# Outputs of a pair in one TensorE visit with the next pair's scores

## What is computed

```
# attention, for each batch and head
for t in range(768):
    state = alpha[t][:, None] * state + outer(k[t], v[t])   # 48 x 48
    y[t] = q[t] @ state
x = y, tokens as rows, heads side by side                    # 3072 x 384
x = square(relu(x @ w_in)) @ w_out                           # first layer
out = silu(x @ w2_in) @ w2_out                               # second layer
```

## Time and profile before

| | |
|---|---|
| median of 3 runs | 881.98 us (881.14 to 882.66) |
| profiled execution: time | 877.95 us |
| its span, first to last instruction | 876.3 us |
| TensorE matmuls busy | 862.5 us, 98% |
| VectorE busy | 541.2 us, 62% |
| ScalarE busy | 437.0 us, 50% |
| GpSimd busy | 104.2 us, 12% |
| granted TensorE clock, mean | 1.000 of 2.4 GHz |

### The profile page before, as it was taken

One profiled execution on the slowest core, in us unless ns is written; L12 is line 12 of the kernel. 1 busy time (PEld: TensorE's weight loads), 2 busy tenths in 40 slices (PEclk: granted clock), 3 DMA queues, 4 the chain that ended last, 5 costly groups with the idle time before them and its releaser, 6 DMA issues.

```text
span 876.3 us, 17615 instructions
## 1 busy us (share of the span) xinstructions
PE 862.5 (98%) x6834; PEld 707.5 (81%) x6834; DVE 541.2 (62%) x1072; ACT 437.0 (50%) x770; POOL 104.2 (12%) x127
## 2 busy tenths in 40 slices
PE   6999989999999999999999999999999999999998
PEld 6777768788878788788888888888888888888898
DVE  7788876777767667664334556556754446766620
ACT  5765544455446445544666744445434436554510
POOL 3453300000000000000354003003030003000000
PEclk9999999999999999999999999999999999999999
DMA  8885434333333332300412352000130000110010
GB/s 171 229 236 126 99 67 120 74 76 103 71 81 87 102 79 67 103 20 13 149 43 71 61 113 78 0 1 1 46 100 0 1 1 1 36 37 1 1 48 28
DMA packets 134203, 60.03 MB, mean 69 GB/s; under 512 B 81824, under 2 KB 129312, under 8 KB 134112
## 3 DMA queue, kind: packets, MB, share of 16 engines
q1 hardware_dynamic: 130800, 58.14, 26.9%
q10 hardware_dynamic: 3312, 0.69, 0.4%
HBM read 45.02 MB, written 9.44 MB: 62 GB/s over the span
## 4 chain that ended last, share of the span: by engine, by line
PE 93%; DVE 4%; issue 1%; ACT 1%; DMA 0%; DVEq 0%; ACTq 0%
PE z_ps L1146 21%; PE h_ps L1132 21%; PE h_ps L1175 20%; PE z_ps L1211 11%; PE jobs L1211 7%; PE jobs L1231 3%; PE jobs L1007 1%; PE jobs L1040 1%; PE jobs L1109 1%; DVE decay L1703 1%; PE jobs L1018 1%; PE jobs L1117 1%; PE h_ps L1231 1%; DVE decay L1688 1%; PE z_ps L1078 0%
## 5 line engine op out<-in xcount | busy, mean ns | idle before, releaser
L1429 ACT ACTIVATE g<-h_ps 128x512 f32<-128x512 f32 x96 | 57.4, 598 | 177.5 <-PE h_ps L1132 175.4
L1523 ACT ACTIVATE sum<-sum 128x512 f32<-128x512 f32 x96 | 60.6, 631 | 137.2 <-DVE sum L1871 111.9
L1810 DVE TENSOR_TENSOR g_lo<-g,g_hi 128x512 fp32r<-128x512 f32 x96 | 67.6, 705 | 85.4 <-ACT g L1435 85.3
L1871 DVE TENSOR_TENSOR sum<-h_ps,sum 128x512 f32<-128x512 f32 x120 | 83.0, 691 | 57.1 <-PE h_ps L1175 54.4
L1132 PE MATMUL h_ps<-x_hi,win_hi 128*128 128x512 f32 x288 | 115.0, 399 | 1.2 <-ACT g L1429 0.8
L1146 PE MATMUL z_ps<-g_hi,wout_hi 128*128 128x512 f32 x282 | 114.4, 406 | 0.0
L1132 PE MATMUL h_ps<-x_hi,win_lo 128*128 128x512 f32 x288 | 112.4, 390 | 0.0
L1132 PE MATMUL h_ps<-x_lo,win_hi 128*128 128x512 f32 x288 | 112.2, 389 | 0.0
L1146 PE MATMUL z_ps<-g_hi,wout_lo 128*128 128x512 f32 x282 | 110.2, 391 | 0.0
L1146 PE MATMUL z_ps<-g_lo,wout_hi 128*128 128x512 f32 x282 | 110.1, 390 | 0.0
L1175 PE MATMUL h_ps<-s_hi,t_hi 128*128 128x512 f32 x264 | 103.0, 390 | 0.2 <-DVE sum L1871 0.2
(11 more groups left out here) (169 smaller groups left out, 1532.8 us busy)
## 6 DMA issues: line engine op xcount, KB each, us to landing
z_scratch<-z_sb SPq DMA_DIRECT2D x18, 256.0 KB, 2.7
pre<-z_scratch SPq DMA_DIRECT2D x18, 256.0 KB, 3.9
v_sb<-in_v SPq DMA_DIRECT2D x44, 96.0 KB, 2.6
out_x<-z_stage SPq DMA_DIRECT2D x80, 48.0 KB, 1.7
nat_a<-in_alpha SPq DMA_DIRECT2D x40, 88.0 KB, 2.3
nat_k<-in_k SPq DMA_DIRECT2D x40, 88.0 KB, 2.4
nat_q<-in_q SPq DMA_DIRECT2D x40, 88.0 KB, 2.2
nat_a<-in_alpha SPq DMA_DIRECT2D x40, 80.0 KB, 2.8
```

Source lines behind the costliest of these rows:

```text
L1429: nc.scalar.activation(g[f % 2][:], h_ps[f % 2][:], ACT.Relu).then_inc(act_made, 1)
L1523: nc.scalar.activation(at[:], at[:], ACT.Silu).then_inc(silu_made, 1)
L1810: nc.vector.tensor_tensor(low, g[f % 2][:], high.bitcast(F32), ALU.subtract).then_inc(g_lo_made, 1)
L1871: nc.vector.tensor_tensor(to[:], h_ps[(PRODUCTS * n + r) % 2][:], other[:], ALU.add).then_inc(summed, 1)
```

## The change

For the first three pairs of each unit from unit 1 on (n = 4, 5, 6, 8, 9, 10, and so on to 22: `beside_scores(n)`, 15 pairs), the output job Y(n) gets the step of S(n + 1), and the list of a step's jobs now begins with Y. So on TensorE, Y(n) and S(n + 1) stand in one visit: L1109, L1117, L1007, L1018. In steps: Y(4) 5 to 7, Y(5) 8 to 10, Y(6) 11 to 13, Y(8) 17 to 18, Y(n) otherwise from 4n - 16 to 4n - 14. Y of the last pair of each unit stays, and so do S, I, A and KQ.

As S now follows at once on a bank that Y used, these Y go to other banks: `h_ps[(F - 1) % 2]` instead of `job_ps[2]`, with `job_ps[0]` as before. That bank was emptied by the ReLU of step F - 1 (new wait on `act_made`) and is next written by the first product of step F + 1, which now waits for `y_copied` of the pair. S no longer waits for `y_copied` where it stands behind Y. Since the two banks don't lie side by side, ScalarE's copy and VectorE's addition become two instructions of 256 columns each. On ScalarE the copies stand ahead of the `kp_t` copy of the same step. On VectorE the additions stand directly behind the masks of S, ahead of the step's `g_lo` subtraction; before, they came last in the step. On SP, the wait for `y_copied`, the repacking DMAs and the value loads move along.

```diff
--- before.py
+++ after.py
@@ -152,8 +152,15 @@
     return 256 * units if units < UNITS else 256 * (units - 1) + LAST_OUT
 
 
+def beside_scores(n):
+
+    return n >= PAIRS and n % PAIRS < PAIRS - 1
+
+
 def stage_step(kind, n):
 
+    if kind == "Y" and beside_scores(n):
+        return stage_step("S", n + 1)
     if n < 2 * PAIRS:
         return {"A": 1, "KQ": 2 if n == PAIRS else 3, "S": 4, "I": 4, "Y": 5}[kind] + 3 * (n - PAIRS)
     if n == 2 * PAIRS:
@@ -208,7 +215,7 @@
 def beside(step):
 
     jobs = BESIDE.get(step, []) if isinstance(step, int) and step >= 0 else []
-    return sorted(jobs, key=lambda j: ("S", "I", "A", "Y", "KQ").index(j[0]))
+    return sorted(jobs, key=lambda j: ("Y", "S", "I", "A", "KQ").index(j[0]))
 
 
 def repack_pieces(place):
@@ -452,7 +459,11 @@
 
 
 
-        first_y, middle_y, later_y = z_ps[1], z_ps[0], (job_ps[2], job_ps[0])
+        first_y, middle_y = z_ps[1], z_ps[0]
+
+        def later_y(n):
+
+            return (h_ps[(stage_step("Y", n) - 1) % 2][:] if beside_scores(n) else job_ps[2], job_ps[0])
         half_i = (job_ps[2], job_ps[1])
 
         half_score = [x[:].rearrange("s b t -> s (b t)")[:, 0:BATCH * HALF] for x in score]
@@ -983,7 +994,7 @@
                 wait(pe, q_scaled, n + 1)
 
                 wait(pe, s_copied, 2 * min(n, PAIRS - 1))
-                if n > PAIRS:
+                if n > PAIRS and not beside_scores(n - 1):
                     wait(pe, y_copied, y_count(n))
                 if n > PAIRS and has_state(n - 1):
                     wait(pe, state_made, n - PAIRS)
@@ -1097,11 +1108,15 @@
                 wait(pe, decayed, n - PAIRS + 1)
 
                 wait(pe, i_copied, PAIRS)
+                if n > PAIRS:
+                    wait(pe, y_copied, y_count(n))
+                if beside_scores(n):
+                    wait(pe, act_made, stage_step("Y", n))
                 v_flat = v_tile(n).rearrange("t b h d -> t (b h d)")
 
                 def to(bank, b, place):
                     rows = slice(0, 64) if b < 2 else head_rows(1)
-                    return later_y[bank][rows, place * HALF:(place + 1) * HALF], 64 if b < 2 else HD
+                    return later_y(n)[bank][rows, place * HALF:(place + 1) * HALF], 64 if b < 2 else HD
                 for half in (0, 1):
                     for b in (0, 2, 1, 3):
                         for h in (0, 1):
@@ -1248,6 +1263,9 @@
                 u, f = divmod(F, NF)
                 if u == 0:
                     wait(pe, w_lo_made, 2 * f + 1)
+                for kind, n in beside(F - 1):
+                    if kind == "Y" and beside_scores(n):
+                        pe.wait_ge(y_copied, y_count(n + 1))
                 first_product(u, u % 2, f, win_hi, win_lo, TILES[-1:] if F < 2 else TILES)
                 if F == 0:
                     i_stage(PAIRS - 1)
@@ -1374,6 +1392,13 @@
                     nc.scalar.activation(y_sb[n % 2][:], first_y[0:ROWS, :], ACT.Copy).then_inc(y_copied, 1)
                     return
 
+                if beside_scores(n):
+                    to = y_sb[n % 2][:].rearrange("p (c k t) -> p k c t", c=BATCH, k=2)
+                    for k in (0, 1):
+                        last = nc.scalar.activation(to[:, k], later_y(n)[k][0:ROWS, UT // 2:].rearrange("p (c t) -> p c t", c=BATCH),
+                                                    ACT.Copy)
+                    last.then_inc(within_copied, 1)
+                    return
                 nc.scalar.activation(y_sb[n % 2][:].rearrange("p (c k t) -> p k c t", c=BATCH, k=2),
                                      y_ps[0:ROWS, :].rearrange("p (k x) -> p k x", k=2)[:, :, UT // 2:].rearrange(
                                          "p k (c t) -> p k c t", c=BATCH), ACT.Copy).then_inc(within_copied, 1)
@@ -1786,6 +1811,12 @@
             def y_stage(n):
 
                 wait(dve, within_copied, n - PAIRS + 1)
+                if beside_scores(n):
+                    for k in (0, 1):
+                        to = y_sb[n % 2][:, k * UT // 2:(k + 1) * UT // 2]
+                        last = nc.vector.tensor_tensor(to, later_y(n)[k][0:ROWS, 0:UT // 2], to, ALU.add)
+                    last.then_inc(y_copied, 1)
+                    return
                 sums = y_sb[n % 2][:].rearrange("p (h x) -> p h x", h=2)
                 nc.vector.tensor_tensor(sums, y_ps[0:ROWS, :].rearrange("p (h x) -> p h x", h=2)[:, :, 0:UT // 2], sums,
                                         ALU.add).then_inc(y_copied, 1)
@@ -1889,6 +1920,10 @@
                 for kind, n in jobs_here:
                     if kind == "S":
                         s_stage(n)
+                for kind, n in jobs_here:
+                    if kind == "Y" and beside_scores(n):
+                        y_stage(n)
+                for kind, n in jobs_here:
                     if kind == "KQ":
                         k_stage(n)
                         if n != 2 * PAIRS:
@@ -1918,7 +1953,7 @@
                         a_scan(n)
                         a_grow(n)
                 for kind, n in jobs_here:
-                    if kind == "Y" and n != 2 * PAIRS - 1:
+                    if kind == "Y" and n != 2 * PAIRS - 1 and not beside_scores(n):
                         y_stage(n)
                 if F in T_STEP:
                     low_t(T_STEP[F])
```

## The result

The changed kernel takes **872.68 us** in the median of 6 runs (872.32 to 874.63), against 881.35 for the kernel before (6 runs, 878.11 to 882.66). The medians are 8.7 us apart. The ratio that all runs give is 0.9918, with an interval of 0.9899 to 0.9936, which is 7.2 us less. Forecast were 4.5 us less, 877.5, in 875.4 to 879.9. The direction was right, the size wrong.

A forecast was written before the change was run, and what follows sets the result against it. TensorE was taken as the bound, with 93% of the chain at full clock. Gains of 3.0 (regular pairs), 0.3 (pairs 4 to 6) and 1.2 (pair 8) make 4.5 us, from 881.98 to 877.5; range 875.4 to 879.9.

The forecast's parts named there:

- Terms 1 and 2: TensorE, Y before S: first, one joined visit saves 0.27 us per pair; second, 11 regular pairs from n = 9 save 3.0.
- the 0.02 for S's four waits: Head of S in a joined visit: waits no longer hidden behind long matmuls cost 0.02 us, at most 0.08.
- The 0.33 that the prediction had beside it: Joined visit, alternative price: if each of two tiling-mode changes drains TensorE, 0.39 less 0.227 each, a pair saves 0.33 us.
- Term 2's slacks: Regular joined steps: next first product has 1.1 us to spare after y_copied, I has 0.6 after the kp_t copy.
- Rival D: I visits of joined steps: kp_t copy too late behind Y's copies on ScalarE, kernel slower at 885.6 us; chance 0.05.
- C: Joined visits: fixed 0.3 us belongs to each operand or bank change and stays; gain only 1.5, 880.5 us; chance 0.08.
- A: Steps 13 to 16: VectorE's row isn't stiff, the whole early 0.84 us reaches step 16; 877.0 to 876.3; chance 0.20.
- B: Step 13: Y(6)'s additions land on VectorE's row, pushing x_lo and step 16 back 0.76 us; 878.6; chance 0.15.
- term 3: Pairs 4 to 6: VectorE's row up to x_lo holds step 16, so only 0.3 us gained, bounds 0 and 0.84.
- Term 4: Pair 8: S(9)'s 2.4 us wait on y_copied goes, a shorter one for q_scaled remains; gain 1.21 us, bounds 1.0 and 1.5.

The follow-up runs named there:

- pair8_only: Changed kernel with the joining cut down to Y(8) with S(9), the other pairs as in the kernel before; median 878.59 us, 0.9977 of before.
- s9_later: Changed kernel with Y(6) left at step 11 and S(9), I(9), Y(8) moved from step 18 to 19; median 872.28 us, 0.9906 of before.
- before_again: The kernel before, run again with no edit; median 881.16 us, 0.9999 of before.
- first_three_only: Changed kernel with only Y(4), Y(5), Y(6) joined; median 879.49 us, 0.9992 of before.
- after_again: The changed kernel, run again with no edit; median 873.15 us, 0.9920 of before.
- pair6_apart: Changed kernel with Y(6) left at step 11, not joined; median 874.14 us, 0.9936 of before.
- late_q9: Changed kernel with VectorE writing the q product of pair 9 three times, lengthening the wait before S(9); median 877.42 us, 0.9961 of before.
- after_s9_later: Changed kernel with S(9), I(9) and Y(8) moved from step 18 to 19, Y(6) still joined; median 872.49 us, 0.9905 of before.
- from_pair9: Changed kernel with only the 11 regular pairs from 9 on joined; median 878.64 us, 0.9971 of before.

## Why the prediction was wrong

*The failed step* is the last one: that the median of the runs, 881.98, "lies 4.0 above it; less 4.5 it gives 877.5". I carried the distance from the profiled execution to the median over as a constant. It wasn't: the median of the changed kernel lies 0.3 below its profiled execution. Forecast against the profiled execution, the sum gave 873.5, and the changed kernel's was 872.96. So of the miss of 4.8, 0.5 is the sum and 4.3 the distance.

What the distance of 4.0 was made of, by the 81 executions of before:
- 1.3 is the scatter of three runs: their median was 881.98, that of the 81 is 880.70.
- 1.4 is the fall of the clock behind the wait that the change shortens: mean 880.62 of all, 879.21 of those not fallen.
- 1.3 is that the profiled execution, 877.95, is faster than the mean of those not fallen; of the 81 only three are below it.

The first would have shown with more runs of before, the second is what the change removes, and of the third the larger part is also gone in the changed kernel (mean 873.28, profiled 872.96).

By the means of all executions: 880.62 less 873.28 is 7.3. Of this, 880.62 less 879.21 is 1.4 for the clock (57 of 81, 2.0 each in the mean). The other 5.9 are the 5.2 of the landmarks and 0.7 that no landmark has. The end of the program can move that much: from the start of the last matmul to the end of the span it is 3.2 us in the traces of before and of the changed kernel, but 4.9 in those of pair8_only and s9_later. VectorE's last copy and the output transfers are left there, and the difference lies behind the issue of the last transfer: 2.1 us to the end in the changed kernel (869.00 to 871.1), 3.8 in pair8_only (873.02 to 876.8). Why they land late in some executions stays open, and so does whether the 0.7 lies there.

*Terms 1 and 2, the joined visit: 0.27 forecast, 0.36 measured; 3.0 and 4.0 for 11.* The mechanism was right and the size outside its bounds (0.19 to 0.33). I took the price of an inner group from the first group of a visit (0.50, 0.52). Inside, a group is cheaper: in the 11 regular joined visits the four groups start 0.50, 0.46 and 0.49 apart in the median, so S's first group takes 0.49 there and 0.51 where it comes first. By 0.47 the fixed part of Y is 1.30 - 0.94 = 0.36. And the 0.02 for S's four waits wasn't paid: the third group starts 0.47 after the second, with the waits between. The 0.33 that the prediction had beside it, from 0.39 less 0.227 twice, was nearer, but also low. Stretches from S(9) to the last Y at full clock: 287.63 in each of four (before, before_again, pair8_only, first_three_only) against 283.63, 283.76 and 283.68 (changed, after_again, pair6_apart).

*Term 2's slacks:* 1.18 and 0.63 measured, 1.1 and 0.6 forecast. Rival D had no ground, and C falls with term 1. Of A and B, which are about term 3, neither came in full: the stretch neither gained the 0.84 of A nor lost the 0.8 of B.

*Term 3, pairs 4 to 6: 0.3 forecast, 0.2 in the mean.* From S(4) to S(8), five traces with Y(4) to Y(6) joined (changed, after_again, late_q9, first_three_only, after_s9_later) need 63.98, 63.85, 63.40, 63.36 and 63.62; before and before_again 63.81 and 63.86. In the profiled execution of the changed kernel itself the term is a loss of 0.2. The forecast's picture holds: masks at 94.00 (forecast 94.04), then the addition waits for ScalarE, and the g_lo subtraction starts at 95.64 (forecast 95.55 to 95.6). VectorE in the changed kernel, step 13 (it answers to the earlier trace rows):

```profile
94.00 0.75 DVE L1772 TENSOR_TENSOR score<-jobs,causal 128x256 f32<-128x256 f32 x2 [1.25 <-PE jobs L1029]
94.96 0.42 DVE L1817 TENSOR_TENSOR y_sb<-h_ps,y_sb 112x256 f32<-112x256 f32 x1 [0.21 <-ACT y_sb L1398]
95.31 0.41 DVE L1817 TENSOR_TENSOR y_sb<-jobs,y_sb 112x256 f32<-112x256 f32 x1
95.64 1.02 DVE L1841 TENSOR_TENSOR g_lo<-g,g_hi 128x512 fp32r<-128x512 f32 x1
96.58 0.34 DVE L1797 TENSOR_TENSOR score<-state,decay 112x192 f32<-112x192 f32 x1
```

GpSimd in the same step (it answers to the earlier trace rows):

```profile
95.08 1.03 POOL L846 TENSOR_TENSOR wout_lo<-wout_raw,wout_hi 128x384 fp32r<-128x384 f32 x1
```

The decay product now takes 0.34 and the g_lo subtraction 1.02 instead, beside GpSimd's block of 95.08 to 96.11: another instruction met the block, as forecast. That GpSimd is the cause was argued from the overlap, and wasn't tried.

*Term 4, pair 8: 1.21 forecast, 1.3 measured,* with S(9) at 122.89 (forecast 122.85). VectorE and TensorE there:

```profile
122.10 0.69 DVE L1760 TENSOR_TENSOR qp<-w_ring,decay 112x512 f32<-112x512 f32 x1
122.89 0.69 PE L1018 MATMUL jobs<-qp,kp 48*64 48x64 f32 x32 [1.33 <-issue]
```

The profile names no releaser, but q ends at 122.79, 0.10 before S(9) starts, and late_q9, in which only q comes later, makes the wait longer; so q is what is late next, as forecast. That 122.85 came so near is partly luck: q ended 0.19 later than forecast, and S(9) followed 0.10 behind it instead of 0.25. What was missing is what the wait costs behind its end. The row on which I leaned, a clock of nine tenths or more in every slice, was of one execution.

The range was a little wider than its own bounds give: 0.19 to 0.33 a pair, 0 to 0.84 and 0.8 of spread make 875.5 to 879.5. The measured 872.68 is outside both.

## What to carry to other kernels

One trace is one execution. Where the runs scatter by more than the change is worth, read what differs among them (here the mean granted clock of each) before adding the profile's distance to the median as a constant. A wait of TensorE of 2.4 us is worth more than its length here, and which step a job stands beside can remove it for nothing. The price of a unit of work inside a stretch is better read from a unit inside: here a group of 32 took 0.50 to 0.52 as the first of a visit and 0.46 to 0.49 behind it.

## What the hardware showed that I had not expected

- After a wait of TensorE of 2.4 us, in a program that is otherwise dense, the mean granted clock was under 0.999 in 57 of 81 executions of one and the same kernel. After one of 1.3 us at the same place it was in none of 30, and without a wait in none of 30. Two traces, of from_pair9 and late_q9, show where: the clock goes to 1.2 GHz late in the wait, at costs of 3.1 us (286.75 against 283.63) and 2.8 (286.45). No trace of before itself caught a fall; that it lies there too is shown by the runs that take the wait away. Of the 57, 42 have a mean clock of 0.998, where the two traced executions have 0.995 and 0.996, so most falls of before are smaller than these two: in the mean one costs 2.0.
- What it costs TensorE to go into the small matmuls and back, 0.36 us, is three quarters of what 32 of them cost inside a visit (0.47 to 0.49).
